# Plain fp32 products in place of three-term split products in a fused attention, Fourier, feed-forward and gate kernel

## What is computed

```python
# attention within hash buckets
mask = q_bucket[:, :, :, None] == k_bucket[:, :, None, :]
scores = np.where(mask, scale * np.matmul(q, k.transpose(0, 1, 3, 2)), -1000000000.0)
attn = np.exp(scores - np.max(scores, axis=-1, keepdims=True))
attn = attn / (np.sum(attn, axis=-1, keepdims=True) + 1e-09)
x = (attn @ v)                                  # laid out as (2, 768, 512)
# Fourier mixing and the network
mixed = np.real(np.fft.fft(np.fft.fft(x, axis=1), axis=2)).astype(np.float32)
u = x + mixed
un = (u - mu) / np.sqrt(var + 1e-06)
x = u + np.maximum(un @ w_ch1, 0.0) @ w_ch2     # 512 -> 2048 -> 512
# gate: causal convolution of 5 taps, value and output products
gate = 1.0 / (1.0 + np.exp(-gate_pre))          # gate_pre = sum_k conv_w[k] * x shifted
out = (gate * (x @ w_val)) @ w_out              # 512 -> 512 -> 512
```

## Time and profile before

| what | value |
|---|---|
| median of 3 runs | 672.47 us |
| span of the profiled execution | 672.3 us |
| PE busy, share of the span | 638.7 us, 95% |
| PE weight loads | 512.0 us, 76% |
| DVE busy | 364.8 us, 54% |
| ACT busy | 307.5 us, 46% |
| POOL busy | 250.7 us, 37% |
| mean granted TensorE clock | 0.990 |
| moved by DMA | 42.08 MB, mean 63 GB/s |

### The profile page before, as it was taken

One profiled execution on the slowest core, in us unless ns is written; L12 is line 12 of the kernel. 1 busy time (PEld: TensorE's weight loads), 2 busy tenths in 40 slices (PEclk: granted clock), 3 DMA queues, 4 the chain that ended last, 5 costly groups with the idle time before them and its releaser, 6 DMA issues.

```text
span 672.3 us, 11293 instructions
## 1 busy us (share of the span) xinstructions
PE 638.7 (95%) x3810; PEld 512.0 (76%) x3810; DVE 364.8 (54%) x599; ACT 307.5 (46%) x586; POOL 250.7 (37%) x202
## 2 busy tenths in 40 slices
PE   2899999999999999888999999999999999996998
PEld 1667576766666675888888888889888888885786
DVE  3878786968778785987211111116333333369720
ACT  2877776868686773355322222223222222251132
POOL 6543333334252341844333333326444444342130
PEclk9999999999999999989999999999999999998899
DMA  5822231324132000100222221520222221000102
GB/s 125 248 71 71 71 94 47 94 68 112 56 91 71 0 25 1 48 1 0 64 63 62 62 62 62 188 63 30 65 62 62 62 62 47 1 0 1 62 32 94
DMA packets 34262, 42.08 MB, mean 63 GB/s; under 512 B 3520, under 2 KB 22208, under 8 KB 34240
## 3 DMA queue, kind: packets, MB, share of 16 engines
q1 hardware_dynamic: 32512, 37.77, 19.6%
q0 software_dynamic: 1728, 4.02, 2.3%
HBM read 38.63 MB, written 3.15 MB: 62 GB/s over the span
## 4 chain that ended last, share of the span: by engine, by line
PE 81%; DVE 11%; issue 3%; POOL 2%; ACT 1%; DMA 1%; SPq 0%; DVEq 0%; POOLq 0%; ACTq 0%
PE banks L1457 20%; PE banks L1445 20%; PE banks L1260 10%; PE banks L1243 10%; PE banks L1307 6%; PE banks L1552 5%; DVE row_min L927 2%; PE banks L1199 2%; PE banks L1536 2%; DVE x_then_u_then_gate L1135 2%; PE banks L1380 2%; PE banks L1432 1%; DVE x_then_u_then_gate L1132 1%; DVE probT L342 1%; DVE k_b L920 1%
## 5 line engine op out<-in xcount | busy, mean ns | idle before, releaser
L1122 DVE SCALAR_TENSOR_TENSOR h_lo<-banks,h_hi 128x512 fp32r<-128x512 f32 x64 | 35.5, 558 | 180.8 <-ACT h_hi L825 180.8
L927 DVE TENSOR_REDUCE row_min<-banks 128x1 f32<-128x768 f32 x96 | 91.3, 956 | 44.9 <-PE banks L1243 44.4
L676 ACT ACTIVATE prob<-banks,row_min 128x768 f32<-128x768 f32 x96 | 87.0, 906 | 30.7 <-DVE row_min L927 30.7
L1445 PE MATMUL banks<-unT_hi,w_hi 128*128 128x512 f32 (+1 forms) x256 | 86.3, 337 | 0.0
L1445 PE MATMUL banks<-unT_hi,w_lo 128*128 128x512 f32 (+1 forms) x256 | 86.2, 337 | 0.0
L1445 PE MATMUL banks<-unT_lo,w_hi 128*128 128x512 f32 (+1 forms) x256 | 86.1, 336 | 0.0
L1307 PE MATMUL banks<-ident,prob 128*128 128x128 f32 x576 | 79.7, 274 | 2.5 <-DVE probT L342 1.5
L501 POOL TENSOR_TENSOR k_b<-k_raw,k_a 64x768 fp32r<-64x768 f32 x16 | 29.2, 1826 | 125.6 <-ACT k_a L659 125.6
L1307 PEld LDWEIGHTS banks<-ident,prob 128*128 128x128 f32 x576 | 67.3, 140 | 10.3 <-ACT probT L342 2.6
L563 POOL TENSOR_TENSOR w_lo<-w_stage,w_hi 128x512 fp32r<-128x512 f32 x32 | 43.6, 1363 | 82.9 <-ACT w_hi L741 82.9
L1260 PE MATMUL banks<-probT,v_in 128*64 128x384 f32 x384 | 72.3, 498 | 0.7 <-ACT outT L686 0.7
(11 more groups left out here) (148 smaller groups left out, 1223.5 us busy)
## 6 DMA issues: line engine op xcount, KB each, us to landing
w_stage<-in_moe_w_ch SPq DMA_DIRECT2D x64, 256.0 KB, 2.9
q_raw<-in_q SPq DMA_DIRECT2D x32, 192.0 KB, 3.3
k_raw<-in_k SPq DMA_DIRECT2D x32, 192.0 KB, 3.6
v_in<-in_v SPq DMA_DIRECT2D x16, 192.0 KB, 2.4
out<-y_out SPq DMA_DIRECT2D x12, 256.0 KB, 2.0
seq_tables_sb<-in_dft POOLq DMA_DIRECT2D x6, 386.0 KB, 3.5
wvo_stage<-in_moe_w_val SPq DMA_DIRECT2D x1, 1024.0 KB, 5.2
wvo_stage<-in_moe_w_out SPq DMA_DIRECT2D x1, 1024.0 KB, 7.9
```

The costliest lines, as they stand in the source:

```text
L676: act.activation(prob[s % 2][:, :, :], s_tile(s), ACT.Exp, bias=row_min[:, s:s + 1], scale=-1.0, accum_out=row_sum[:, s:s + 1]).then_inc(e ...
L927: dve.tensor_reduce(row_min[:, s:s + 1], s_tile(s), AX.XY, ALU.min).then_inc(min_ready, 1)
L1122: dve.scalar_tensor_tensor(out=h_lo[:, slot, at:at + size], in0=h_bank[c], scalar=0.0, in1=h_hi[:, slot, at:at + size].bitcast(F32), op0=A ...
L1445: op = pe.matmul(h_bank[c], w_[:, slot, kb, :], x_[:, kb, at:at + size], start=(kb == 0 and m == 0), stop=(kb == KB - 1 and m == 2))
```

## The change

All products of the network, the values and the outputs are made as one plain fp32 matmul on unsplit fp32 tiles. Every hi and lo tile of these stages and every instruction that made one is gone; the split products of the scores and of the Fourier stage stay. The weights go from DMA straight into four buffers (`W_SLOTS`), and PE waits for the DMA itself. The values are made in two halves of 384 columns out of `x2`, where they were made in chunks of 512 and 256 out of the split copy. `ffn1` and `ffn2` keep their order.

```diff
+    W_SLOTS = 4
-        w1_stage = sb("w1_stage", [P, 2, KB, P])
-        w1_hi = sb("w1_hi", [P, 2, KB, P], F32R)
-        w1_lo = sb("w1_lo", [P, 2, KB, P], F32R)
+        w1_sb = sb("w1_sb", [P, W_SLOTS, KB, P])
+        w2_sb = sb("w2_sb", [P, W_SLOTS, DM])
...
             def load_w(n, f, slot):
-                need(sp, w1_lo_done, n - 1)
-                sp.dma_start(w1_stage[:, slot, :, :], w1_v[f]).then_inc(w1_loaded[slot], 16)
+                need(sp, h_full, 2 * n - (2 * W_SLOTS - 2))
+                sp.dma_start(w1_sb[:, slot, :, :], w1_v[f]).then_inc(w1_loaded[slot], 16)
+                need(sp, ffn2_done, n - (W_SLOTS - 1))
+                sp.dma_start(w2_sb[:, slot, :], w2_v[f]).then_inc(w2_loaded[slot], 16)
-            load_w(0, 0, 0)
-            load_w(1, 1, 1)
+            for f in range(W_SLOTS):
+                load_w(f, f, f)
...
-            split_w1(0, 0)
-            split_w1(1, 1)
-            split_w2(0, 0)
...
-                    act.copy(un_hi[b][:, :, cols], src[:, :, rows]).then_inc(unT_hi_done, 1)
+                    act.copy(unT[b][:, :, cols], src[:, :, rows]).then_inc(unT_done, 1)
...
-                    act.activation(h_hi[:, slot, at:at + size], h_bank[c], ACT.Relu).then_inc(h_hi_done, 1)
+                    act.activation(h_sb[:, slot, at:at + size], h_bank[c], ACT.Relu).then_inc(h_done, 1)
...
-                act.copy(un_hi[b][:, :, :].rearrange("p k (c n) -> p (k c) n", c=2),
-                         x2[b][:, :, PAD:PAD + HALF]).then_inc(x2_hi_done, 1)
...
-                    act.copy(gv_hi[:, d, :], gate(b)[:, d * S:(d + 1) * S]).then_inc(gv_hi_done, 1)
...
             def gate_values(b, d):
                 dve.wait_ge(gate_ready, b + 1)
-                for c, (at, size) in enumerate(CH):
+                for c in range(2):
                     dve.wait_ge(val_full, 2 * (b * KB + d) + c + 1)
-                    dst = gate(b)[:, d * S + at:d * S + at + size]
-                    dve.tensor_tensor(dst, PS[:, VAL_BANKS[d][c], 0:size], dst, ALU.mult).then_inc(gv_done, 1)
+                    at = d * S + c * HALF
+                    dst = gate(b)[:, at:at + HALF]
+                    dve.tensor_tensor(dst, PS[:, VAL_BANKS[d][c], 0:HALF], dst, ALU.mult).then_inc(gv_done, 1)
...
                     for kb in range(KB):
-                        for m, (w_, x_) in enumerate(((w1_hi, un_hi[b]), (w1_lo, un_hi[b]), (w1_hi, un_lo[b]))):
-                            op = pe.matmul(h_bank[c], w_[:, slot, kb, :], x_[:, kb, at:at + size],
-                                           start=(kb == 0 and m == 0), stop=(kb == KB - 1 and m == 2))
+                        op = pe.matmul(h_bank[c], w1_sb[:, slot, kb, :], unT[b][:, kb, at:at + size],
+                                       start=(kb == 0), stop=(kb == KB - 1))
...
-                    for w_, h_ in ((w2_hi, h_hi), (w2_lo, h_hi), (w2_hi, h_lo)):
-                        for c, (at, size) in enumerate(CH):
-                            op = pe.matmul(acc(d, c), w_[:, slot, cols], h_[:, slot, at:at + size], start=False,
-                                           stop=last, skip_group_check=True)
+                    for c, (at, size) in enumerate(CH):
+                        op = pe.matmul(acc(d, c), w2_sb[:, slot, d * P:(d + 1) * P], h_sb[:, slot % 2, at:at + size],
+                                       start=False, stop=last, skip_group_check=True)
...
             def values(b, d):
+                for c in range(2):
                     for kb in range(KB):
+                        op = pe.matmul(PS[:, VAL_BANKS[d][c], 0:HALF], wvo[:, kb, d * P:(d + 1) * P],
+                                       x2[b][:, 2 * kb + c, PAD:PAD + HALF], start=(kb == 0), stop=(kb == KB - 1))
...
             def output(b, t, blocks):
-                    pe.wait_ge(gv_lo_done, KB * b + d + 1)
-                    for m, (g_, w_) in enumerate(((gv_hi, wvo_hi), (gv_lo, wvo_hi), (gv_hi, wvo_lo))):
-                        op = pe.matmul(PS[:, OUT_BANKS[b][t], :], g_[:, d, rows], w_[:, KB + d, :],
-                                       start=(d == 0 and m == 0), stop=(d == KB - 1 and m == 2))
+                    pe.wait_ge(gv_done, 2 * (KB * b + d) + 2)
+                    op = pe.matmul(PS[:, OUT_BANKS[b][t], :], gate(b)[:, at:at + P], wvo[:, KB + d, :],
+                                   start=(d == 0), stop=(d == KB - 1))
```

More of the change, by code:

```diff
@@ L735, in _, with copy_unT @@
             pair(NP, 2)
[L737 to L743, removed]
-                act.wait_ge(w2_loaded[slot], 16 * loads)
-                need(act, ffn2_done, n - 1)
-                act.copy(w2_hi[:, slot, :], w2_stage[:, slot, :]).then_inc(w2_hi_done, 1)
[L748 to L753, removed]
+            def copy_unT(n):
                 b, t = tile_at(n)
@@ L1149, in _ @@
             dve.wait_ge(taps_spread, 2)
-            with dve.Fori(0, FB // 2) as j:
-                for u in range(2):
-                    relu_lo(2 * j + u, u)
             take_x2(0)
@@ L1156, in _ @@
             dve.wait_ge(x2_lead, B + 1)
-            with dve.Fori(0, FB // 2) as j:
-                relu_lo(FB + 2 * j, 0)
-                conv_tap(0, j, 0)
-                conv_tap(0, j, 1)
-                relu_lo(FB + 2 * j + 1, 1)
-                for tap in range(2, TAPS):
-                    conv_tap(0, j, tap)
+            with dve.Fori(0, 2 * KB) as m:
+                for tap in range(TAPS):
+                    conv_tap(0, m, tap)
             take_x2(1)
@@ new lines, in ffn_rounds @@
+            def ffn_rounds(b):
+                first = b * FB // W_SLOTS
+                with pe.Fori(first + 1, first + FB // W_SLOTS) as j:
+                    ffn1(W_SLOTS * j, b, 0, j + 1)
+                    ffn2(W_SLOTS * j - 1, W_SLOTS - 1, j)
+                    for u in range(1, W_SLOTS):
+                        ffn1(W_SLOTS * j + u, b, u, j + 1)
+                        ffn2(W_SLOTS * j + (u - 1), u - 1, j + 1)
+                ffn2(FB * (b + 1) - 1, W_SLOTS - 1, first + FB // W_SLOTS, True)
@@ L1506, in _ @@
                     open_acc(1, d, c)
-            with pe.Fori(0, FB // 2 - 1) as j:
-                ffn1(FB + 2 * j + 1, 1, 1)
-                ffn2(FB + 2 * j, 0, False)
-                ffn1(FB + 2 * j + 2, 1, 0)
-                ffn2(FB + 2 * j + 1, 1, False)
-            ffn1(2 * FB - 1, 1, 1)
-            ffn2(2 * FB - 2, 0, False)
-            ffn2(2 * FB - 1, 1, True)
+            for u in range(1, W_SLOTS):
+                ffn1(FB + u, 1, u, FB // W_SLOTS + 1)
+                ffn2(FB + u - 1, u - 1, FB // W_SLOTS + 1)
+            ffn_rounds(1)
             def values(b, d):
```

207 lines of the change are left out of this document (47 added, 160 removed).

## The result

The change made the kernel slower: 737.12 us (median of 4 runs, 736.85 to 737.32) against 673.13 us for the kernel before on the same chip, a ratio of 1.0947 (95% interval 1.0928 to 1.0966). The profiled execution has a span of 735.5 us against 672.3.

What follows compares the result with a forecast made beforehand. PE was taken to bound the kernel, busy 95% of the span. Span 672.3 + 75.4 (network) + 10.0 (gate stage) - 5.8 (Fourier stage) = 751.9, so 752 us, with a range of 738 to 768.

Steps and rivals of the forecast that it cites:

- PE bounds the network, so the freed engines give nothing there.: Network: the chain is gapless matmuls on PE, so removing copies on ACT, DVE or POOL gives nothing by itself.
- One plain product is two records, one record two passes.: All changed products: a plain fp32 product takes four passes, against three for the split.
- I take 0.875, between the two measured values.: Price in ns per column and record, chosen between 0.859 from `open_acc` and 0.888 from P x V; network +75.4 us.
- A record costs its columns alone ... 2.5 ns per record would make it 735.: Rival for plain products: 0.833 ns per column, 731 us, or 735 by the skill's rule; chance 0.08.
- 0.833 and 0.888: Ends of the price in ns per column and record: columns alone at 2.4 GHz, and the value from P x V.
- a third of the way to 731: Low end of the forecast range, set at 738 us, towards the 731 of records costing their columns alone.
- Gate stage: Values, gate products and outputs: PE never waits once POOL's instructions go; stage 86.0 us against 76.0, +10.0.
- Fourier stage, -5.8: Fourier stage and way into the network: gains from removed weight splits and low parts, -5.8 us, ends -3 and -8.
- About -1.2: Fourier stage: us gained when POOL's three weight splits no longer stand beside DVE's L1086, 1.71 us there against 0.48.
- -4.6: Ahead of the network: us gained by removing DVE's low parts, seven taken at 0.65 together.
- Weights and early loads, nothing.: Weight loads at the start and in the loop: no cost expected; the other end at the start is one landing, 2.9 us.

Runs made afterwards that it cites:

- Experiment 1: Kernel before with ffn1 and ffn2 as one plain fp32 product, all split copies and subtractions kept, gate stage untouched: 735.67 us, ratio 1.0917.
- experiment 3: Kernel before with the network's hi and lo tiles in fp16, three products kept: 654.04 us; then stationary operands cut to 127 columns: 654.8 us.
- experiment 5: Kernel before with the gate stage's low parts moved from POOL to DVE, and batch 0's gate products and sigmoid ordered earlier: 662.99 us, ratio 0.9858.

## Why the prediction was wrong, point by point

- **PE bounds the network, so the freed engines give nothing there.** Right. Experiment 1 keeps all their work and is 61.3 us longer all the same.
- **One plain product is two records, one record two passes.** Right: 16 records per phase, and four records of one head take as long as eight of two.
- **"I take 0.875, between the two measured values."** This is the step that failed. The measured price is 5.16 us / 6144 = 0.840 ns per column and record, its columns at 2.4 GHz plus 2.5 ns per record. The 0.888 came from dividing a whole group by its rounds, which spread the 0.15 us of entering and leaving a narrow tiling over 8 of them; the steady 0.32 us was already in the kernel before's trace. The 0.859 from `open_acc` was a step of 0.110 us that even a 1-column record needs, as the prediction itself remarked. Both "measured values" were thus upper bounds, and the middle of two upper bounds was taken. On 491,520 column-records the 0.035 ns make 17.2 us, more than the whole miss of 16.4 on the span. That the median lies only 0.9 us outside the range is luck in part: adding 0.2 us for the distance of time and span, where the runs have 1.6, took 1.5 off.
- **"A record costs its columns alone ... 2.5 ns per record would make it 735."** This rival came true, at 735.5, and had got 0.08. The prediction had dismissed the rule of the Trainium skill, "TensorE: Matmul & The Clock Gate", Part 1, because fp32r's rows contradict it (4.21 us a phase against 3.9). The trace agrees with the rule for fp16, where the phase is 3.90, and for plain records if their columns are counted twice and the 2.5 ns once; it disagrees for fp32r alone. A row of another type was used to throw out a rule for this one.
- **The range.** "0.833 and 0.888" held the price, but the low end was cut at "a third of the way to 731", at 738, for a case to which the nearest steady row, the 0.32 us between rounds, pointed.
- **Gate stage.** Mechanism right, PE never waits and the clock stays up; +6.5 for +10.0 by the same price: 8 x 5.16 + 48 x 0.858 = 82.5. The tap that took 7.00 us beside POOL takes 0.41.
- **Fourier stage, -5.8.** Measured -5.4. "About -1.2" for the casts was right: 16.40 less 15.20. "-4.6" for the low parts was 4.2, and about 1.1 of that was the clock, a term that the prediction didn't have; as a price of the low parts alone it was too high.
- **Weights and early loads, nothing.** Right: no wait on a load stands ahead of any phase, and the attention ended within 0.3 us of before.

## What to carry to other kernels

A plain fp32 matmul is four passes and a three-term split is three, so plain fp32 lost where TensorE set the time, however much work it spared the other engines. Three terms in fp16 beat both here, where the data fit fp16's range: each pass costs its columns and little more. When a price is read from a trace, take the distance between starts in the middle of a long run; a group's time divided by its count also contains what the group pays once, and a step that doesn't shrink with size is a floor and no price.

## What the runs showed of the hardware that was not expected

- An fp32r matmul costs 231 ns for 512 columns. A two-byte one costs 216, and a record of a plain one also only 2.5 ns beyond its columns. 7% of the network's time (268.7 us against 64 x 3.90) was paid for the operand type.
- Products on different parts of the array ran side by side even with four records of one head queued ahead of the other's (1.45 us for 8 either way). Alternating them in the program gained nothing.
- Going from full-width to 64-column products and back costs about 0.15 us each time.
- The weight load of a two-byte operand takes 98 ns for 128 columns and 138 for 127 (the 0.10 and 0.14 of experiment 3). The Trainium skill, "TensorE: Matmul & The Clock Gate", Weight-path perf modes, ties the fast load to 128 weights that are not fp32; the rows agree. Neither load was on the path, though the longer one takes more time than the 109 ns from one 256-column matmul to the next.
- DVE's three casts took 1.71 us beside POOL's subtractions of 3.75 us, 0.98 beside those of 3.03, and 0.49 with POOL idle.
- The granted clock fell to 0.50 in the Fourier stage of the kernel before and stayed at 1.00 in experiment 5, which has the same instructions there. The fall cost about 1.1 us.
